# First attention block loaded and transposed in groups of two and four tiles, with mask tables built in three steps

## What is computed

```python
n_global, n_local = 8, 96                      # read from device memory by the kernel
scores = q @ k.T / sqrt(64)
rel = pos[:, None] - pos[None, :]
is_global = pos[None, :] < n_global
is_local = (rel >= 0) & (rel < n_local)
dist = where(is_global & ~is_local, n_local, abs(rel))
scores = where(is_global | is_local, scores - slope[h] * dist, -1e9)
a = exp(scores - max(scores)); a = a / (sum(a) + 1e-9)
x = a @ v                                       # then router + 8 experts, then 4 dense experts
```

## Time and profile before

| | us |
|---|---|
| median of 3 runs | 790.16 |
| the three runs | 790.33, 777.43, 790.16 |
| the profiled execution, device time | 778.11 |
| its span, first to last instruction | 776.4 |
| TensorE busy in it | 743.0 (96%) |
| DVE busy | 471.6 (61%) |
| ACT busy | 329.1 (42%) |
| POOL busy | 42.2 (5%) |

### The profile page before, as it was taken

How to read it: one execution, slowest core, us unless ns; L and a number is a source line. 1 busy time by engine, 2 the same in 40 slices (tenths; PEclk the granted TensorE clock), 3 DMA queues, 4 the chain that set the end, 5 groups by cost and what they waited for, 6 DMA issues and landing times.

```text
span 776.4 us, 11260 instructions
## 1 busy us (share of the span) xinstructions
PE 743.0 (96%) x4199; PEld 661.5 (85%) x4199; DVE 471.6 (61%) x924; ACT 329.1 (42%) x586; POOL 42.2 (5%) x86
## 2 busy tenths in 40 slices
PE   3999999699999879999999999999999999999998
PEld 2889889488888778998989989989889899898896
DVE  5766666699888587654573475275365265456442
ACT  2666566388988352521432333234144043143230
POOL 3100100110100410000000000000000000000000
PEclk9999999699999999999999999999999999999999
DMA  9569970599990530030021011002003003000112
GB/s 152 101 152 247 291 217 21 199 394 390 390 389 35 156 130 1 1 109 1 0 71 39 1 55 54 1 17 92 0 0 108 0 0 109 0 0 0 41 41 81
DMA packets 86944, 79.28 MB, mean 102 GB/s; under 512 B 50802, under 2 KB 56948, under 8 KB 86900
## 3 DMA queue, kind: packets, MB, share of 16 engines
q1 hardware_dynamic: 81540, 71.32, 29.6%
q0 software_dynamic: 1600, 5.24, 2.2%
q10 hardware_dynamic: 3760, 2.14, 0.9%
HBM read 70.30 MB, written 8.39 MB: 101 GB/s over the span
## 4 chain that ended last, share of the span: by engine, by line
PE 89%; DVE 6%; DMA 2%; issue 1%; ACT 1%; POOL 0%; DVEq 0%; SPq 0%; POOLq 0%
PE ps L1881 32%; PE ps L1858 30%; PE ps L1761 11%; PE ps L1585 3%; PE ps L1610 2%; PE ps L1609 2%; PE ps L1594 2%; PE ps L1565 2%; PE ps L1626 1%; PE ps L1618 1%; PE ps L1736 1%; DVE xs L1448 1%; DVE X L1105 1%; PE ps L1817 1%; DVE ql L1065 1%
## 5 line engine op out<-in xcount | busy, mean ns | idle before, releaser
L1858 PE MATMUL ps<-xs,w1s 128*128 128x384 f32 x1344 | 237.7, 336 | 0.0
L1881 PE MATMUL ps<-w2s,h_hi 128*128 128x512 f32 x768 | 237.1, 390 | 0.6 <-DVE X L1486 0.6
L1858 PEld LDWEIGHTS ps<-xs,w1s 128*128 128x128 f32 x1344 | 235.1, 189 | 1.3
L1881 PEld LDWEIGHTS ps<-w2s,h_hi 128*128 128x128 f32 x768 | 143.7, 188 | 30.2 <-DVE X L1486 1.0
L1881 PE MATMUL ps<-w2s,h_lo 128*128 128x512 f32 x384 | 149.7, 390 | 0.0
L1488 DVE SCALAR_TENSOR_TENSOR X<-ps,prn,X 128x512 f32<-128x512 f32 x84 | 63.1, 751 | 121.7 <-PE ps L1881 121.3
L953 ACT ACTIVATE shared<-ps 128x384 f32<-128x384 f32 x96 | 46.1, 488 | 157.5 <-PE ps L1858 157.3
L1457 DVE TENSOR_TENSOR shared<-ps,shared 128x384 f32<-128x384 f32 x96 | 53.4, 557 | 93.6 <-PE ps L1858 93.3
L1881 PEld LDWEIGHTS ps<-w2s,h_lo 128*128 128x128 f32 x384 | 72.1, 188 | 15.0
L956 ACT ACTIVATE h_hi<-shared 128x384 fp32r<-128x384 f32 x96 | 50.5, 527 | 67.7 <-DVE shared L1457 67.7
L1023 DVE TENSOR_TENSOR piece_lo<-ring,piece_hi 128x1024 fp32r<-128x1024 f32 x48 | 56.4, 1220 | 5.4 <-ACT piece_hi L775 5.4
(11 more groups left out here) (183 smaller groups left out, 798.3 us busy)
## 6 DMA issues: line engine op xcount, KB each, us to landing
ring<-in_moe_w SPq DMA_DIRECT2D x24, 1024.0 KB, 12.3
raw<-in_moe_w SPq DMA_DIRECT2D x16, 1024.0 KB, 5.1
shared<-in_moe_w SPq DMA_DIRECT2D x8, 1024.0 KB, 10.7
X<-in_k SPq DMA_DIRECT2D x16, 192.0 KB, 4.3
shared<-in_q SPq DMA_DIRECT2D x16, 192.0 KB, 4.3
X<-in_v SPq DMA_DIRECT2D x16, 192.0 KB, 3.1
x_d<-X SPq DMA_DIRECT2D x8, 384.0 KB, 3.2
X<-x_d SPq DMA_DIRECT2D x2, 1536.0 KB, 16.5
```

The costliest lines, as they stand in the source:

```text
L1858: mm = pe.matmul(out_, w1s[:, wp, WI[name], c, f * P:(f + 1) * P], xs[:, 3 * b:3 * b + 3, xp, XI[name], c, :], start=(not onto and x == 0 ...
L1881: mm = pe.matmul(ps[:, 6 + k % 2, :], h_, w2s[:, wp, c, :], start=(x == 0 and c == 0), stop=(x == 2 and c == 3))
```

## The change

For block 0 only, the groups are cut at tile 2: `k0` and `q0` hold tiles 0 and 1, `k1` and `q1` the tiles 2 to 5. The first two tiles have loads of their own (64 KB a head), k's on SP ahead of the rest and q's on ACT's queue; the three small loads move from ACT to the end of SP's list. TensorE transposes `k0` and `q0`, and ACT copies them out, before either reads the flag. The other two groups follow after the branch, still ahead of `scores(0)`. `windows` of block 0 comes in two pieces with the global columns between, and TensorE waits for them at units 1 and 3, no longer at unit 0. In block 0 the groups of block 1 are filled at units 2 to 5 instead of 0 to 3.

The mask tables take three DVE steps (`distances`) instead of eight, on tables that POOL has partly prepared. The 128 columns of `ONE` are made ahead of the branch; the 256 columns `PREV` and `OWN`, with their `head_bias` for two heads, after `masked(0)`. The flag takes seven DVE steps instead of eleven. ACT runs one Exp on a constant at the start. The six further heads' tables are made one in each block (at i = 4). `keys_low(0, 1)` and `queries_low(0, 1)` come after `masked(1)`.

```diff
-        FIRST = ["k0", "k1", "q0", "q1"]
+        FIRST = ["k0", "q0", "k1", "q1"]
+        def tiles(n, c):
+            cut = 2 if n == 0 else 4
+            return range(0, cut) if c == 0 else range(cut, NI)
+        def filled(u):
+            n, i = u // NI, u % NI
+            x = i - 2 if n == 0 else i
+            if n + 1 < NB and 0 <= x < 4:
+                return n + 1, ("k0", "k1", "q0", "q1")[x]
...
 sync:
-            for b in range(2):
-                load_k(0, b)
-                load_q(0, b)
-                load_v(0, b)
+            first = part_of(0, 0)
+            for hh in range(2):
+                sp.dma_start(kn[0][:, first, hh * D:(hh + 1) * D], heads(k, 0, 0)[hh][:, first, :]).then_inc(ld_first[0], 16)
+            load_k(0, 0, part_of(0, 1))
+            load_q(0, 0, part_of(0, 1))
+            load_v(0, 0)
+            load_k(0, 1)
+            load_q(0, 1)
+            load_v(0, 1)
+            sp.dma_start(wg9[:, :, 0:E], w_gate.rearrange("(k p) e -> p k e", p=P)).then_inc(ld_small, 16)
+            with nc.allow_non_contiguous_dma(reason="512 elements"):
+                sp.dma_start(wg9[:, :, E], w_skip.rearrange("(k p) -> p k", p=P)).then_inc(ld_small, 16)
+            sp.dma_start(pr[:, :, :], probs.rearrange("(t p) e -> p t e", p=P)).then_inc(ld_small, 16)
...
@@ gpsimd @@
-                for n in range(NB):
-                    windows(n)
+                cut = tiles(0, 1)[0]
+                pool.wait_ge(k_lo, 1)
+                windows(0, 1, cut + 1)
+                globals_(0)
+                pool.wait_ge(k_lo, 2)
+                windows(0, cut + 1, NI)
...
@@ scalar @@
+            for hh in range(2):
+                act.dma_start(qn[0][:, first, hh * D:(hh + 1) * D], heads(q, 0, 0)[hh][:, first, :]).then_inc(ld_first[1], 16)
+            act.wait_ge(bounds, 1)
+            act.activation(nn[0:1, 15:16], nn[0:1, 10:11], ACT.Exp).then_inc(act_on, 1)
...
+            keys_high(0, 0)
+            queries_high(0, 0)
+            f = banded(act)
             with act.If(f > 0):
-                for c in range(2):
-                    keys_high(0, c)
-                for c in range(2):
-                    queries_high(0, c)
+                keys_high(0, 1)
+                queries_high(0, 1)
...
@@ vector @@
+            def distances(s, after):
+                dve.tensor_scalar(far_key[:, s], key[:, s], nn[:, 0:1], -NEG, ALU.is_ge, ALU.mult).then_inc(setup, 1)
+                dve.tensor_scalar(dist[:, s], past[:, s], nn[:, 1:2], None, ALU.min).then_inc(setup, 1)
+                dve.wait_ge(setup, after + 2)
+                dve.scalar_tensor_tensor(barred[:, s], past[:, s], nn[:, 1:2], far_key[:, s], ALU.is_ge, ALU.mult).then_inc(setup, 1)
+                dve.wait_ge(setup, after + 3)
+            dve.wait_ge(const_p, 10)
+            distances(slice(ONE, ONE + P), 0)
             f = banded(dve)
...
-                table(rel, key, in_win, t_a, t_b, dist, step)
-                dve.memset(lg, 0.0).then_inc(setup, 1)
-                for c in range(2):
-                    keys_low(0, c)
-                for c in range(2):
-                    queries_low(0, c)
-                for h in range(2):
-                    head_bias(h)
+                keys_low(0, 0)
+                queries_low(0, 0)
+                for h in range(2):
+                    head_bias(h, slice(ONE, ONE + P))
                 for u in range(NU_):
                     n, i = u // NI, u % NI
                     masked(u)
+                    if u == 0:
+                        distances(slice(PREV, BW), 5)
+                        for h in range(2):
+                            head_bias(h, slice(PREV, BW))
+                    if u == 1:
+                        keys_low(0, 1)
+                        queries_low(0, 1)
...
-                    if n == 0 and 2 + i < H:
-                        head_bias(2 + i)
+                    if i == 4 and 2 + n < H:
+                        head_bias(2 + n)
...
@@ tensor @@
-            pe.wait_ge(const_p, 17)
-            f = banded(pe)
+            pe.wait_ge(const_p, 3)
...
-                if i == 0:
-                    pe.wait_ge(kw_done, 4 * n + 4)
-                if i in (0, 4):
-                    pe.wait_ge(q_lo, 2 * n + i // 4 + 1)
+                for c in range(2):
+                    if i == tiles(n, c)[0]:
+                        pe.wait_ge(k_lo, 2 * n + c + 1)
+                        pe.wait_ge(q_lo, 2 * n + c + 1)
+                if u == 1:
+                    pe.wait_ge(kw_done, 4)
+                elif u == tiles(0, 1)[0] + 1:
+                    pe.wait_ge(kw_done, 6)
+                elif i == 1:
+                    pe.wait_ge(kw_done, 4 * n + 6)
...
-            pe.wait_ge(ld_small, 48)
+            fill(0, "k0")
+            fill(0, "q0")
+            f = banded(pe)
             with pe.If(f > 0):
-                for g in FIRST:
-                    fill(0, g)
+                fill(0, "k1")
+                fill(0, "q1")
                 pe.wait_ge(v_ones, 4)
```

More of the change, by code:

```diff
@@ L323, in build @@
         bias_ready = sem("bias_ready")
+        bounds = sem("bounds")
+        act_on = sem("act_on")
+        ld_first = [sem(f"ld_first_{g}") for g in "kq"]
         ld_q = [sem(f"ld_q{j}") for j in range(2)]
@@ L481, in build, with part_of @@
         LG = 400
-        FIRST = ["k0", "k1", "q0", "q1"]
-        FILL = FIRST + [None, None]
-        groups = [(0, g) for g in FIRST]
[L485 to L490, removed]
+        FIRST = ["k0", "q0", "k1", "q1"]
+        def tiles(n, c):
+            cut = 2 if n == 0 else 4
+            return range(0, cut) if c == 0 else range(cut, NI)
+        def part_of(n, c):
+            return slice(tiles(n, c)[0], tiles(n, c)[-1] + 1)
+        def filled(u):
[3 more added lines that the diff above has]
+                return n + 1, ("k0", "k1", "q0", "q1")[x]
+            return None
+        groups = [(0, g) for g in FIRST]
+        for u_ in range(NU_):
+            n_, i_ = u_ // NI, u_ % NI
+            if filled(u_):
+                groups.append(filled(u_))
+            if n_ and i_ in (0, 3):
+                groups.append((n_ - 1, "xa" if i_ == 0 else "xb"))
         groups += [(NB - 1, "xa"), (NB - 1, "xb")]
@@ L786, in keys_high @@
                     act.wait_ge(s_done, NI * (n - 1))
-                act.activation(kh[n % 2][:, tiles(c), P:2 * P], group(n, f"k{c}", c), ACT.Copy).then_inc(k_hi, 1)
+                act.activation(kh[n % 2][:, part_of(n, c), P:2 * P], group(n, f"k{c}", c), ACT.Copy).then_inc(k_hi, 1)
             def queries_high(n, c):
@@ L792, in queries_high @@
                     act.wait_ge(s_done, NI * (n - 1))
-                act.activation(qh[n % 2][:, tiles(c), :], group(n, f"q{c}", c), ACT.Copy, scale=-0.125).then_inc(q_hi, 1)
+                act.activation(qh[n % 2][:, part_of(n, c), :], group(n, f"q{c}", c), ACT.Copy, scale=-0.125).then_inc(q_hi, 1)
             def xo_out(n, half):
@@ L1562, in transposed @@
                 bank_free(place[n, g])
-                pe.wait_ge(loaded[n % 2], (n // 2) * 32 + 32)
-                for x, t in enumerate(range(4 * c, min(4 * c + 4, NI))):
+                if (n, c) == (0, 0):
+                    pe.wait_ge(ld_first["kq".index(g[0])], 32)
+                else:
+                    pe.wait_ge(loaded[n % 2], (n // 2) * 32 + 32)
+                for x, t in enumerate(tiles(n, c)):
                     mm = pe.transpose(ps[:, bank, x * P:(x + 1) * P], src[n % 2][:, t, :], ident[:, :])
@@ L1622, in logits @@
                 pe.wait_ge(xo_cp, 2 * n + 1 + half)
+                if not half and not n:
+                    pe.wait_ge(ld_small, 48)
                 if not half:
@@ L1636, in _ @@
                     scores(u)
[L1637 to L1638 removed]
+                    if filled(u):
+                        fill(*filled(u))
                     if u >= 1:
```

146 lines of the change are left out of this document (76 added, 70 removed).

## The result

| | before | after |
|---|---|---|
| median, 20 runs each, us | 778.88 | 773.8 |
| lowest, us | 777.43 | 771.89 |
| ratio after/before, 95% interval | | 0.995, 0.9928 to 0.9972 |
| profiled execution, us (span) | 778.11 (776.4) | 773.82 (771.9) |

A forecast was written before the change was run, and what follows sets the result against it. TensorE, busy 743.0 of 776.4 us, was taken as the bound, leaving only the start: 5.1 us gained at `masked(0)`, 3.8 at `scores(2)`, 2.3 at `scores(6)`. Span 774.1 plus 1.7 around it gave 775.8 us, range 772 to 789.

The forecast's parts named there:

- What bounds the kernel: Whole kernel: TensorE busy 743.0 of 776.4 us, so only the start before the first score matmul at 16.00 can gain.
- Flag and branch: Start: seven steps instead of eleven finish the flag at about 6.4, 0.6 us earlier; ACT's moved table load costs nothing.
- DVE ahead of `scores(0)`: DVE at the start: enters the branch at 8.2, low parts done at 9.05, two 128-column `head_bias` by 9.6 us.
- q's second part: Transfer for `q1`: lands at 9.8 us, bounds 8.8 and 11.0, so `scores(0)` starts at 10.9 instead of 16.00.
- DVE between `masked(0)` and `scores(2)`: First block, DVE: about 4.7 us puts `scores(2)` at 16.7 instead of 20.52, cutting gain from 5.1 to 3.8 us.
- TensorE from `scores(2)` on: First block to `scores(6)`: gain left is 0.2 to 4.3 us by when the clock rises; 2.3 us taken.
- Steady blocks: Later blocks: `head_bias` at i = 4 is covered on DVE and costs nothing; uncovered, six would cost 3.8 us.
- the case that I held likeliest: Whole kernel: gain of 1 to 4 us from the earlier start, range 774 to 777.5 us; chance 0.45.
- the 0.38 that I gave to 782 to 789: Whole kernel: chance of one or two longer low-clock stretches, or a median from the slower kind of run near 790.
- The longer low-clock stretch: Behind attention: one more stretch costs 6.8 us, giving 782.6, two 789; chance 0.38, shared with slower-kind runs.
- Nothing gained: Start: q landing at 11.0 and dearer DVE steps leave no gain, time 778 to 780 us; chance 0.10.
- Full gain: Start: TensorE's clock high at `scores(2)` and low DVE prices gain 4.3 to 5 us, 773 to 774; chance 0.07.

## Why the prediction was right in its range and short in its number

Point by point, in the prediction's order.

**What bounds the kernel: right.** The start alone changed, the blocks and dense stages did not, TensorE's busy time is the same (742.8 us).

**Flag and branch: right.** 6.15 + 0.16 = 6.3 for the flag (6.4). DVE comes out of its branch at 8.12 (8.2). The table load is at 1.85, hidden.

**DVE ahead of `scores(0)`: right.** `queries_low(0,0)` is done at 8.9 (9.05).

**q's second part: the step that failed.** I wrote "I take 9.8", with 8.8 to 11.0 as bounds; it landed at 8.0 or before, sooner than both. Its two transfers in after (the line of q's rest, count and issue times, then issue to landing):

```profile
L569 SPq DMA_DIRECT2D shared<-in_q x2: 508/553/598, 3.8 to 4.3; - x2
...
DMA to landing us min/median/max: 3.6/3.7/3.7
```

3.7 us where it had been 6.0 to 6.6. With the small loads back on ACT's queue the same two take 5.1 to 5.5, which puts their landing at 9.8, the figure that I took, and TensorE's start on them at 9.89: the term was right for a kernel in which the small loads stay. The reasoning "the bytes that must have come by then are the same" counted bytes. The transfer engines' time was the thing to count, and 19.6% of it went into pieces that carry 42 KB. I had named that ACT's queue held them in the trace of before, and then only asked what q's tiles would do in that place, not what their going would give. q's transposes started at 8.25 instead of 9.8, 1.6 us sooner, and took 0.1 less than I had put; together this made `scores(0)` 1.7 too late (10.9 against 9.24). The loads of the small weights were costed by when they are needed ("nothing") and not by what they had been costing.

**DVE between `masked(0)` and `scores(2)`: right in kind, 0.4 too dear.** From 10.31 to the end of `queries_low(0,1)` at 14.55 it took 4.24 us where I had 4.7: `masked(0)` 0.42 (0.6), the five steps 1.85 (1.9), `masked(1)` 0.68 (0.8), the two low parts 1.29 (1.4). Back-to-back steps on DVE overlap by about 0.07 us each, which I had put in for some and not for others. `scores(2)` still waits for DVE: [2.06 <-DVE ql L1121]. The two errors together, 1.7 and 0.4, put `scores(2)` at 16.7 instead of 14.65.

**TensorE from `scores(2)` on: right.** From 5.87 gained at `scores(2)`, 1.29 went by `scores(6)`; I had 1.5 (3.8 to 2.3). One unit was fully slow at 3.59 (3.58 forecast), the next partly at 2.90, then 2.42 and 2.19 (2.57 and 2.28). The spread that I gave to this term (0.2 to 4.3) was too wide by far: the five profiles without constant matmuls whose `scores(2)` lies within 0.5 us of the changed kernel's have `scores(6)` between 25.14 and 25.75, 10.4 to 11.4 us behind it.

**Steady blocks: right.** `head_bias` at i = 4 costs nothing: 100.09 us from `scores(6)` to the last unit's scores, against 100.11.

**The sum.** 2.3 + 1.7 (q) + 0.4 (DVE) + 0.2 (TensorE) = 4.6, against 4.58 at `scores(6)` and 4.5 in the span. The measured median lies in the stated range, 772 to 789, but not in the 774 to 777.5 of the case that I held likeliest. Most of the range's width was there for the kind of run at 790, and the 0.38 that I gave to 782 to 789 met no run of after.

**Rivals.** The longer low-clock stretch didn't show in the profile of after (13.7 us against 13.6); its runs at 778 to 782 may be that or something else. "Nothing gained" rested on q landing late, the wrong direction. "Full gain" is what happened, but not for its reason: I had tied it to a high clock at `scores(2)`, and the clock was low there (0.58 for the pair at 14.65); the gain came from earlier starts. Its chance of 0.07 was too small because the range of q's landing had no side for "sooner than any row of today", and a transfer's landing when others leave its engines is just such a value.

**What I had no price for.** Of the two things that name the change, the runs show the groups of two tiles to be neutral; of the tables, three steps instead of eight gain, and making the first 128 columns first doesn't. That the fills of block 1 move by two units looked like bookkeeping, and the run with the tables alone shows a wait that it avoids: 1.40 us of TensorE for block 1's k, 0.62 with the small loads moved. What the move is worth by itself no run shows.

## What to carry to other kernels

Cost a moved transfer on both sides: what it delays where it goes, and what it frees where it was; in the transfer view, packets and share of time say it, bytes don't. Splitting the first group smaller brings the first result forward and puts the rest of that group's work in front of a later one; follow it to the third or fourth unit before counting it. Where an engine's clock depends on its work, idle time at the start is paid twice, and constant matmuls at the start and in the gaps gave 2.3 us and more at `scores(6)` here, some 1.6 to 2.5 us of the span.

## What the hardware showed that I had not expected

The 2,608 packets of some 16 bytes on ACT's queue took 19.6% of the transfer engines' time from 2 to 10 us for 0.04 MB. They delayed SP's transfers, by 0.7 us for k's first tiles (TensorE's first transposes at 6.49 instead of 5.76) and by 1.3 to 1.6 us for q's rest and for block 1's k. Two more issues on SP in front of q's rest delayed what waits for it by 0.10 us, not 0.98: SP's issuing wasn't the limit. In two runs transposes alone brought TensorE to 2.4 GHz, and idle times of 1.45 and 2.29 us in thinly used stretches were followed by the low level; with seven matmuls in the second gap it stayed high over the 1.18 us left.
